# Weight sums of an expert step on VectorE, the weight split two chunks later, and a new order of loads around the FFN

## What is computed

```python
q_p, k_p = phi(q), phi(k)                  # exp(+-(x @ w_phi - max|.|)), 256 features
num = q_p @ (k_p.T @ v); den = q_p @ k_p.sum(tokens) + 1e-6
x = (num / den)                            # [2304, 512]
e_idx = argmax(x @ w_gate)                 # one of 8 experts for each token
out[mask] = gate_w * eom[mask, e] * (relu(x[mask] @ w1[e]) @ w2[e])
xn = out / sqrt(mean(out * out) + 1e-6) * rms_g
g = xn @ w_gate                            # 512 -> 1536
y = (silu(g) * (xn @ w_val)) @ w_out       # 1536 -> 512
```

## Time and profile before

| | us |
|---|---|
| median of 3 runs (885.47 to 888.86) | 886.7 |
| the profiled execution | 884.25 |
| its span | 882.5 |
| attention, steps 0 to 7, FFN up, FFN out: TensorE's start of each | 0, 210.5, 451.5, 731 |
| TensorE busy | 845.0 |
| VectorE, ScalarE, GpSimd busy | 527.9, 347.9, 186.9 |
| mean granted TensorE clock, share of full speed | 0.985 |

### The profile page before, as it was taken

One profiled execution on the slowest core, in us unless ns is written; L12 is line 12 of the kernel. 1 busy time (PEld: TensorE's weight loads), 2 busy tenths in 40 slices (PEclk: granted clock), 3 DMA queues, 4 the chain that ended last, 5 costly groups with the idle time before them and its releaser, 6 DMA issues.

```text
span 882.5 us, 16593 instructions
## 1 busy us (share of the span) xinstructions
PE 845.0 (96%) x6216; PEld 764.6 (87%) x6217; DVE 527.9 (60%) x912; ACT 347.9 (39%) x548; POOL 186.9 (21%) x190
## 2 busy tenths in 40 slices
PE   8999999999979899999989999999999989999997
PEld 6686858678978899999978989999999988888886
DVE  5688888997555743445478777666765665122220
ACT  4555445662246333332254443333433433222211
POOL 1010303023263443424530031111110000111101
PEclk9999999999999899999999999999999999999999
DMA  8613714021647346554673852232222944343330
GB/s 284 205 55 151 257 53 161 2 77 35 261 166 221 136 132 144 103 126 138 179 175 126 275 182 78 78 79 78 78 78 58 390 161 167 131 143 112 128 107 36
DMA packets 65370, 122.41 MB, mean 139 GB/s; under 512 B 9216, under 2 KB 43136, under 8 KB 62496
## 3 DMA queue, kind: packets, MB, share of 16 engines
q1 hardware_dynamic: 57744, 91.98, 34.3%
q0 software_dynamic: 3488, 17.85, 5.3%
q10 hardware_dynamic: 4080, 11.80, 3.8%
HBM read 77.54 MB, written 44.09 MB: 138 GB/s over the span
## 4 chain that ended last, share of the span: by engine, by line
PE 78%; DVE 10%; DMA 5%; issue 5%; ACT 1%; POOL 0%; DVEq 0%; SPq 0%; POOLq 0%; ACTq 0%
PE ps L1220 9%; PE ps L1222 8%; PE ps L1221 8%; PE ps L1273 5%; PE ps L1271 5%; PE ps L1272 5%; PE ps L1128 3%; PE ps L1141 3%; PE ps L1129 3%; PE ps L1130 3%; PE ps L1142 3%; PE ps L1143 3%; PE ps L969 3%; PE ps L1024 3%; PE ps L929 2%
## 5 line engine op out<-in xcount | busy, mean ns | idle before, releaser
L1220 PE MATMUL ps<-sH,tb 128*128 128x384 f32 x504 | 171.8, 341 | 9.4 <-DVE val L2009 4.9
L1222 PE MATMUL ps<-sH,tb 128*128 128x384 f32 x504 | 170.6, 338 | 0.0
L1221 PE MATMUL ps<-sL,tb 128*128 128x384 f32 x504 | 170.6, 338 | 0.0
L1220 PEld LDWEIGHTS ps<-sH,tb 128*128 128x128 f32 x504 | 95.5, 190 | 12.4 <-DVE val L2009 6.6
L1221 PEld LDWEIGHTS ps<-sL,tb 128*128 128x128 f32 x504 | 95.7, 190 | 0.1
L1222 PEld LDWEIGHTS ps<-sH,tb 128*128 128x128 f32 x504 | 95.6, 190 | 0.0
L2027 DVE TENSOR_TENSOR hTL<-h_st,hTH 128x768 fp32r<-128x768 f32 x36 | 32.9, 954 | 97.4 <-ACT hTH L1528 97.4
L1128 PE MATMUL ps<-xmH,w1H 128*128 128x288 f32 x256 | 78.3, 306 | 13.2 <-DVE hmL L1796 9.3
L1796 DVE SCALAR_TENSOR_TENSOR hmL<-ps,hmH 128x288 fp32r<-128x288 f32 x64 | 29.1, 454 | 94.2 <-ACT hmH L1376 93.7
L1273 PE MATMUL ps<-woH,hTL 128*128 128x512 f32 x216 | 84.1, 389 | 0.0
L1272 PE MATMUL ps<-woL,hTH 128*128 128x512 f32 x216 | 84.1, 389 | 0.0
(11 more groups left out here) (245 smaller groups left out, 1772.4 us busy)
## 6 DMA issues: line engine op xcount, KB each, us to landing
h_dram<-hid SPq DMA_DIRECT2D x36, 384.0 KB, 2.7
h_st<-h_dram SPq DMA_DIRECT2D x18, 768.0 KB, 4.2
t_dram<-tb SPq DMA_DIRECT2D x6, 1792.0 KB, 5.7
t_raw<-in_ffn_up SPq DMA_DIRECT2D x13, 512.0 KB, 3.3
tb<-t_dram ACTq DMA_DIRECT2D x6, 1024.0 KB, 7.9
xin<-xs_dram SPq DMA_DIRECT2D x9, 578.2 KB, 9.0
xs_dram<-zrow SPq DMA_DIRECT2D x8, 578.2 KB, 7.9
qT<-in_q SPq DMA_DIRECT2D x4, 1152.0 KB, 5.7
```

The source lines that it names most:

```text
L1220: e.matmul(to, wh, xh, start=(fresh and c == 0), stop=False, skip_group_check=True)
L1221: e.matmul(to, wh, xl, start=False, stop=False, skip_group_check=True)
L1222: done = e.matmul(to, wl, xh, start=False, stop=(c == 1), skip_group_check=True)
```

## The change

- **Step:** `weight_sums` moves from GpSimd to VectorE, behind `relu_low` of chunk 0. `weights_high` moves on ScalarE from chunk 0 to chunk 2, behind the expert pieces; `weights_low` on VectorE from chunk 1 to chunk 3.
- **First set:** in the early case SyncE issues the load of set 1 before it waits for the scatter.
- **Token numbers:** `numbers_out` is a helper of its own. For the step before the last it is called at unit 8, for the last at unit 10. The last rows' load (`group_in(2)`) comes at unit 4 rather than 5.
- **First units:** VectorE makes the first high part `sH[0][0]` itself; GpSimd's squares of the last step wait for seven low parts.
- **Out weights:** loaded in two halves, the first at unit 20, the second at the end of group 0 (unit 28), where before all of it was loaded in thirds. Their splits begin at unit 30 and are two at a time.

```diff
-OUT_HIGH_AT = {(31, "C"): (0,), (32, "A"): (1, 2, 3), (33, "A"): (4, 5, 6), (34, "A"): (7, 8, 9), (35, "A"): (10, 11)}
-OUT_LOW_AT = {(32, "A"): (0,), (32, "B"): (1, 2), (33, "A"): (3,), (33, "B"): (4, 5), (34, "A"): (6,), (34, "B"): (7, 8),
-              (35, "A"): (9,), (35, "B"): (10, 11)}
-TILE0_HIGH_AT = {(34, "C"): 0, (35, "C"): 1}
-TILE0_LOW_AT = {(35, "A"): 0, (35, "C"): 1}
+OUT_HIGH_AT = {(30, "C"): (0, 1), (31, "A"): (2, 3), (31, "C"): (4,), (32, "A"): (5, 6), (33, "A"): (7, 8),
+               (34, "A"): (9, 10), (34, "C"): (11,)}
+OUT_LOW_AT = {(31, "A"): (0, 1), (31, "B"): (2,), (32, "A"): (3, 4), (32, "B"): (5, 6), (33, "B"): (7, 8),
+              (34, "B"): (9, 10), (35, "A"): (11,)}
+TILE0_HIGH_AT = {(35, "A"): 0, (35, "C"): 1}
+TILE0_LOW_AT = {(35, "B"): 0, (35, "C"): 1}
...
-        wo_st = piece(0, 8)("wo_st", [P, NF, DM])
+        wo_st = [placer(at_raw, 12288)("wo_st0", [P, NF // 2, DM]), piece(0, 4)("wo_st1", [P, NF // 2, DM])]
...
-        hT_put = [placer(at_raw, 12288), piece(0, 4)]
+        hT_put = [piece(4, 4), placer(at_raw, 12288)]
...
             e.wait_ge(s["tab_set"], 2)
             e.wait_ge(s["pe_P"], B * 2 * NS)
             e.wait_ge(s["c_pad"], 16 * E)
+            with e.If(early > 0):
+                e.sem_inc(s["e_in"], 16)
+                e.sem_inc(s["e_st"], 32)
+                step_weights_in(1)
             e.wait_ge(s["scat"], 16 * B * NJ)
...
             with e.Fori(0, total - 2) as n:
                 rows_next(n + 2)
                 weights_out(n + 1)
                 step_weights_in(n + 2)
-                rows_out(n)
+                col, row = column_of(n), row_of(n)
+                rows_out(n, col)
+                numbers_out(n, col, row)
...
             group_in(0)
-            rows_out(prior)
+            prior_col, prior_row = column_of(prior), row_of(prior)
+            rows_out(prior, prior_col)
...
                 if u == ROOT_AT + 1:
-                    e.wait_ge(s["dve_xn"], total + 1)
-                    settle(e, "carry_sp")
-                    e.dma_start(xn_dram[:, :, bass.ds(last_col, G)], x2g[:, :, :]).then_inc(s["xst"], 16)
-                if u == ROOT_AT + 2:
+                    rows_out(last, last_col)
                     e.wait_ge(s["s_lo"], 7)
                     e.wait_ge(s["xst"], total * 16 + 32)
                     settle(e, "carry_sp")
...
                 if u == 8:
...
+                    numbers_out(prior, prior_col, prior_row)
+                if u == 10:
+                    numbers_out(last, last_col, last_row)
...
+                if u == 20:
+                    e.wait_ge(s["s_lo"], 7 * NSG)
+                    e.wait_ge(s["s_add"], 8)
+                    e.dma_start(wo_st[0][:, :, :], ffn_out[:, 0:NF // 2, :]).then_inc(s["wo_in0"], 16)
                 if u == last_of_group(0):
                     e.wait_ge(s["pe_D"], u + 1)
-                    for third in range(3):
-                        e.dma_start(wo_st[:, third * 4:third * 4 + 4, :], ffn_out[:, third * 4:third * 4 + 4, :])\
-                            .then_inc(s[f"wo_in{third}"], 16)
+                    e.dma_start(wo_st[1][:, :, :], ffn_out[:, NF // 2:NF, :]).then_inc(s["wo_in1"], 16)
...
             def step(par, g):
-                weight_sums(g)
                 add_squares(g - 1)
                 gate_rows(g + 1)
...
             row_sums(0, 1)
+            e.wait_ge(s["s_lo"], 7)
             add_squares(total - 1)
...
                     if m == 0:
                         copy_out(g - 1)
-                        weights_high(g)
                     if split is not None:
                         for n in PIECES_AT.get(m, ()):
                             split(n)
+                    if m == 2:
+                        weights_high(g)
...
-            for o in range(4):
+            for o in range(1, 4):
                 row_high(0, o)
...
+            def weight_sums(g):
+
+                e.wait_ge(s["e_in"], g * 16 + 16)
+                settle(e, "carry_dve")
+                e.tensor_tensor(t_raw[2][:, 4:6, :, :], t_raw[2][:, 1:3, :, :], t_raw[2][:, 0:2, :, :], ALU.subtract)\
+                    .then_inc(s["e_add"], 1)
+                e.wait_ge(s["e_add"], g * 3 + 1)
+                settle(e, "carry_dve")
+                e.tensor_tensor(t_raw[2][:, 1, :, :], t_raw[2][:, 2, :, :], t_raw[2][:, 4, :, :], ALU.subtract)\
+                    .then_inc(s["e_add"], 1)
+                e.wait_ge(s["e_add"], g * 3 + 2)
+                settle(e, "carry_dve")
+                e.tensor_tensor(t_raw[2][:, 6, :, :], t_raw[2][:, 3, :, :], t_raw[2][:, 1, :, :], ALU.subtract)\
+                    .then_inc(s["e_add"], 1)
...
-                    if m == 1:
+                    if m == 0:
+                        weight_sums(g)
+                    if m == 3:
                         weights_low(g)
...
+            e.wait_ge(s["x_in0"], 16)
+            e.wait_ge(s["pe_s1"], total * FC)
+            settle(e, "carry_dve")
+            e.tensor_copy(sH[0][0][:, :, :], xst[0][:, 0:2, 0:GN]).then_inc(s["s_hi0"], 1)
             for o in range(4):
                 row_low(0, o)
```

63 lines of the change are left out of this document (22 added, 41 removed).

## The result

The changed kernel takes 874.77 us (median of 4 runs, 871.70 to 876.78) where the kernel before, run on the same chip, takes 887.78 (885.47 to 890.02). The ratio is 0.9851, 95% interval 0.9808 to 0.9893: faster by 1.5%, or 13.0 us. The forecast was 871.4, range 866 to 881. The profiled execution took 873.63 us, with a span of 871.9.

What follows compares the result with a forecast made beforehand. TensorE, busy 845.0 of 882.5 us, bounds the kernel; gains come only where it is idle or slow. Terms sum to -15.3 us from 884.25, giving 868.95; 2.45 added for the median makes 871.4 us, range 866 to 881.

Steps and rivals of the forecast that it cites:

- Step 1: Expert step 1: TensorE's wait of 3.40 us falls to 1.7, that of 1.22 to about 0.3; -2.6 us.
- the turn: Calm steps: whether VectorE's second sum or GpSimd's squares issue first; VectorE assumed first by 0.05 us, 0.1 us each.
- Step 2: Expert step 2: waits of 1.98 and 2.73 us mostly go, with a 3.1 us slow stretch; -6.0 us.
- The cover: Calm steps: the next set's load, issued later, still lands before VectorE wants it, with 7 us to spare.
- Calm steps: Expert steps 3 to 7, without TensorE waits before: VectorE's sums add 0.1 us each; +0.5 us.
- Rival 1: GpSimd's squares go before VectorE's second sum: 1.45 instead of 0.1 us in six steps, +8.1 us, 879.5; 28%.
- Rival 2: GpSimd's squares go first and each gap brings a slow clock stretch: +13.5 us, 893.0, slower than before; 5%.
- Last step and first units: End of expert loop and first FFN units: shorter collision -0.8, low operands in time -2.7, group's rows earlier -0.3 us.
- The wait for the group's rows: First FFN units: moving the token numbers brings the rows earlier; of 1.81 us about 1.5 are left, -0.3 us.
- The three low operands: First FFN units: TensorE's waits of 0.92, 0.92 and 0.87 us for low operands go; -2.7 us.
- Units 8 to 10: FFN units: last group's load goes out earlier, so the wait of 2.01 us moves rather than goes; +0.5 us.
- units 29 to 33: FFN units: loading half the out weights early removes the 2.49 us wait and 1.4 us of slow clock; -3.9 us.

Runs made afterwards that it cites:

- its second: Second profile of the changed kernel, timed again with no edit: median 870.87 us, ratio 0.9841 to the kernel before.
- the last one: Changed kernel plus row store ahead of the load, token numbers behind the gather, squares behind the sums, first operand on GpSimd: 868.53 us, ratio 0.9801.

## Why the prediction was right, and where it was not

**Step 1 (-2.6; measured -4.1).** Right in mechanism, too small in size. The wait at chunk 3 was put at 1.7 us; it is none. The forecast let the first sum wait for the load until 244.1. The load had landed when VectorE came: first sum at 247.86, or 243.5 on the clock of before, 0.6 us earlier, and the second sum began 0.02 us ahead of the squares, which lost the turn there too. That is luck as much as foresight: with the turn lost the wait is 1.30 us, near the forecast. The slow stretch behind the old wait (granted clock 0.51 from 251.60 to 255.00 us), which the forecast left in, went with it.

**Step 2 (-6.0; measured -3.7).** The sum is the right one for what it counted: with the row store's wait removed, by moving it or by moving the token numbers, step 2 takes 29.15 or 29.09 us, 5.9 or 6.0 less than the 35.09 of before. The failed step is "the later split also delays the set's store ... and with it the next load ... covered by 7 us". The chain was followed to the load and not to the store of the rows, which is next in the same queue and had 0.1 us of slack; its wait of 3.40 us on ScalarE and 1.83 on TensorE is what the runs show in place of the missing gain. The cover itself was there in the calm steps: the load is issued 5.4 us later there and nobody waits for it.

**Calm steps (+0.5; measured +0.8).** The turn goes as forecast, the squares are 0.28 us longer (0.2 forecast), the third sum takes 2.10 us. There is no wait, since the low part of chunk 1 starts 3.8 us behind that of chunk 0 and not 4.3; each step is 0.2 us longer all the same, and 27.22 us again where the squares wait for the sums or the sums are on GpSimd.

**Rival 1 (28%).** Its price was right, 1.26 us of waiting and 1.5 us a step over the kernel before, and its condition too: the order of issue decides, at 0.10 us. The Trainium skill (SBUF — State Buffer, Who interferes with whom) says that issue order decides who blocks; both traces agree. That the changed kernel was on the right side by 0.01 to 0.02 us is luck, as the prediction's "thin" says.

**Rival 2 (5%).** In those gaps the clock stays at 1.00. Length alone is not what decides: behind 1.83 us in step 2 of the changed kernel's first profile the clock stays at 1.00, behind 1.78 us in step 3 of its second it falls to 0.57, and behind 2.25 us in step 2 of that one to 0.65.

**Last step and first units (-0.8, -2.7, -0.3; measured -3.7 to unit 3).** The sum is right, the parts are not. The last step's wait fell from 1.58 to 0.60 in the first profile and is 1.86 in the second, so the gain of 0.8 us is not shown. The wait for the group's rows fell from 1.81 with its slow stretch to 0.50 in both: the small transfer was the clog, and taking it away was worth more than the -0.3 given to it (1.9 us when it is put back). The three low operands are in time, but VectorE's first operand comes 3.21 us late out of the loop, and 2.52 us with a slow stretch stand at the start instead. The prediction had VectorE begin as soon as its semaphores allowed. The Trainium skill (DMA: Bandwidth & Descriptors, Why small descriptors are slow) gives an overhead of about 3 cycles per packet, by which the numbers would hold nothing up. The trace speaks against going by that alone: the 4-byte packets take 9 ns each in its records, and what stands behind them is held for microseconds.

**Units 8 to 10 (+0.5; measured -0.5), and units 29 to 33 (-3.9; measured -4.4).** The wait of 2.01 became 1.54. The DMA term is confirmed by taking the early load away. Between units 20 and 28 the early half costs nothing that can be told: that stretch takes 58.68 to 59.67 us in profiles with it, 58.68 and 59.63 in the two without.

## What to carry to other kernels

A transfer that lands just in time shows in no view of waits. Before something in a queue is moved, list everything behind it in that queue, with the time when it lands and the time when it is wanted; here the slack was 0.1 us, and it cost 2 to 6 us. Look at the other engines' queues too: a store issued just behind another queue's 2 MB load sent its first packet 4.4 us after its issue. Put a transfer of many tiny pieces where nothing follows it soon. And ask of a change with several parts which part pays: the one that its title names first paid nothing that could be measured.

## What the runs showed of the hardware

A transfer of 288 pieces of 4 bytes, HBM to HBM, 1.1 KB in all, slows what stands around it for 5 to 9 us: 52 GB/s with single 2056-byte packets of up to 5.6 us, against 227 GB/s and 0.23 us with the transfer elsewhere. The store just ahead of it is reported late too: its last packet ended at 275.97 us, and the engine that waited for it started at 280.87. With another transfer between the two, the report follows the last packet by 0.4 to 0.5 us.

Where two queues asked for large transfers at nearly the same time, the order of issue went with the delay, in the one profile that has the other order: 1.22 us behind a 2 MB load of another queue, a 1.8 MB store sent its first packet 4.4 us after its issue and took 12.6 us; 0.27 us ahead of that load, 0.9 and 8.0 us.

When VectorE's subtraction and GpSimd's product both read SBUF, the one issued first goes first: 0.01 us ahead, and the 128x256 subtraction takes 0.43 us; 0.10 us behind, and it takes 2.29.

The clock does not follow from the length of a gap alone. The same wait of 1.95 us at the same line, in the kernel with the token numbers moved and in the last one:

```profile
518.00:522.00 4.00, 4.00 (x16) 0.66 0.28 85
```

```profile
515.30:519.30 4.00, 4.00 (x23) 1.00 0.30 84
```

16 matmuls in 4 us against 23, and 7 matmuls at 0.174 us are 1.2 us. That is most of the 1.6 us by which the way from unit 9 to unit 12 differs in the two, 25.70 against 24.13. Over all profiles this way takes 23.6 to 24.5 us where the clock stays up and 25.5 to 26.2 in the six where it falls there.
